# A new order of expert groups and of the last products, with the carried state updated on VectorE

## What is computed

```
C = f_stab * C + i_stab * outer(v_t, k_t);   n = f_stab * n + i_stab * k_t
y_t = sigmoid(o_t) * (C @ q_t) / max(|n . q_t|, 1)
x = y, heads side by side, 1536 x 320
out = sum over 4 experts e of  p[:, e] * (relu(x @ w1[e]) @ w2[e])     # 320 -> 1024 -> 320
```

## Time and profile before

| | |
|---|---|
| median of 3 runs | 412.25 us |
| the profiled execution, its own time | 412.83 us |
| span of its profile | 410.9 us |
| mean granted clock of TensorE | 0.996 of full |
| instructions | 7284 |
| busy: TensorE / VectorE / ScalarE / GpSimd | 403.0 / 261.8 / 192.0 / 193.2 us |
| idle of TensorE in the span | 7.9 us |

### The profile page before, as it was taken

One profiled execution on the slowest core, in us unless ns is written; L12 is line 12 of the kernel. 1 busy time (PEld: TensorE's weight loads), 2 busy tenths in 40 slices (PEclk: granted clock), 3 DMA queues, 4 the chain that ended last, 5 costly groups with the idle time before them and its releaser, 6 DMA issues.

```text
span 410.9 us, 7284 instructions
## 1 busy us (share of the span) xinstructions
PE 403.0 (98%) x2650; PEld 389.8 (95%) x2650; DVE 261.8 (64%) x490; ACT 192.0 (47%) x378; POOL 193.2 (47%) x227
## 2 busy tenths in 40 slices
PE   8999999999899999999999999999999999999997
PEld 8899999999899999999999999979999999999997
DVE  5885786759444538346249893668665666667654
ACT  4575478659242548434125442344553345434420
POOL 4865835487940558821602001567435643556300
PEclk9999999999899999999999999999999999999999
DMA  7889929684970606341016002222012211230002
GB/s 265 283 283 391 381 92 346 234 284 159 369 274 2 225 2 228 116 176 48 2 30 140 0 2 83 85 84 85 12 73 83 83 29 57 83 101 17 0 2 96
DMA packets 18052, 54.48 MB, mean 133 GB/s; under 512 B 2177, under 2 KB 8850, under 8 KB 16866
## 3 DMA queue, kind: packets, MB, share of 16 engines
q1 hardware_dynamic: 17442, 52.63, 36.8%
q10 hardware_dynamic: 576, 1.40, 1.0%
HBM read 50.40 MB, written 2.05 MB: 128 GB/s over the span
## 4 chain that ended last, share of the span: by engine, by line
PE 94%; DVE 4%; issue 1%; ACT 0%; POOL 0%; DVEq 0%
PE acc_ps L1611 21%; PE hid_ps L1592 21%; PE acc_ps L1677 16%; PE out_ps L1548 5%; PE hid_ps L1677 3%; PE acc_ps L1592 2%; PE out_ps L1655 2%; PE out_ps L1656 2%; PE out_ps L1654 2%; PE out_ps L1653 2%; PE out_ps L1555 2%; PE hid_ps L1441 1%; PE score_ps L1492 1%; PE score_ps L1655 1%; PE add_ps L1655 1%; PE add_ps L1656 1%
## 5 line engine op out<-in xcount | busy, mean ns | idle before, releaser
L1149 DVE SCALAR_TENSOR_TENSOR h_lo<-hid_ps,h_hi 128x384 fp32r<-128x384 f32 (+1 forms) x70 | 35.9, 513 | 84.6 <-ACT h_hi L809 84.3
L809 ACT ACTIVATE h_hi<-hid_ps 128x384 fp32r<-128x384 f32 (+1 forms) x70 | 31.8, 455 | 108.6 <-PE hid_ps L1592 108.5
L1611 PE MATMUL acc_ps<-w_hi,h_hi 128*128 128x320 f32 x208 | 66.4, 319 | 2.5 <-DVE y_acc L1169 2.2
L1611 PE MATMUL acc_ps<-w_hi,h_lo 128*128 128x320 f32 x208 | 64.4, 310 | 0.0
L1611 PE MATMUL acc_ps<-w_lo,h_hi 128*128 128x320 f32 x208 | 64.2, 308 | 0.0
L1592 PE MATMUL hid_ps<-xt_hi,w_hi 128*128 128x384 f32 (+1 forms) x210 | 57.1, 326 | 0.1
L1592 PE MATMUL hid_ps<-xt_hi,w_lo 128*128 128x384 f32 (+1 forms) x210 | 56.6, 324 | 0.0
L612 POOL TENSOR_TENSOR w_lo<-w_raw,w_hi 128x384 fp32r<-128x384 f32 x40 | 45.1, 1131 | 23.5 <-ACT w_hi L795 23.4
L682 POOL TENSOR_TENSOR w_hi<-w_raw,w_hi 128x640 fp32r<-128x640 f32 x12 | 19.6, 1634 | 53.1 <-ACT w_hi L852 53.1
L1611 PEld LDWEIGHTS acc_ps<-w_hi,h_hi 128*128 128x128 f32 x208 | 39.5, 190 | 2.8 <-DVE h_lo L1149 2.7
L676 POOL TENSOR_TENSOR left_lo<-w_raw,left_hi 128x384 fp32r<-128x384 f32 x12 | 13.2, 1101 | 56.6 <-ACT left_hi L835 56.6
(11 more groups left out here) (251 smaller groups left out, 996.6 us busy)
## 6 DMA issues: line engine op xcount, KB each, us to landing
w_raw<-in_w_b SPq DMA_DIRECT2D x19, 704.0 KB, 7.3
w_raw<-in_w_s SPq DMA_DIRECT2D x12, 832.0 KB, 4.6
raw<-in_qk_s SPq DMA_DIRECT2D x8, 1024.0 KB
g_all<-g_dram SPq DMA_DIRECT2D x10, 512.0 KB, 6.9
kv<-in_kv_n SPq DMA_DIRECT2D x12, 352.0 KB, 6.1
q_pack<-in_q_p SPq DMA_DIRECT2D x10, 192.0 KB, 6.9
out_y<-y_acc SPq DMA_DIRECT2D x12, 160.0 KB, 1.8
carry<-g_dram SPq DMA_DIRECT2D x30, 60.0 KB
```

The lines of the kernel that those rows point to most:

```text
L809: nc.scalar.activation(h_hi[:, M % RING, 0:cols], hid_bank(M)[:, 0:cols], ACT.Relu).then_inc(hid_hi, 1)
L1149: nc.vector.scalar_tensor_tensor(h_lo[:, M % RING, 0:cols], hid_bank(M)[:, 0:cols], 0.0, h_hi[:, M % RING, 0:cols].bitcast(fp32), ALU.max, ...
L1611: last = nc.tensor.matmul(acc_ps[t][:, 0:DM], x, w, start=(f == 0 and i == 0), stop=(f == NF - 1 and i == 2))
```

## The change

The second and third visit of the first expert are swapped with the third expert (`LOADS`, `GROUPS`): expert 2 meets units 0 to 5 in slots 24 to 39 (three units at a time), and expert 0 meets units 2 and 3 in slots 40 to 47. `EARLY` drops to 24, `DN_END` to 24, and the start slots of units 5 to 10 and the slots of `CAST` and `SUB` move. `carry_state` leaves GpSimd's queue and becomes three `scalar_tensor_tensor` operations of VectorE on 120x123 elements, in the same slot T0+6. In the wide steps, step 1 gets the order 1, 6, 7, 4, 2, 5, 3 with its four downs behind the second, third, fourth and sixth product, the last step gets 4 ahead of 2, and ScalarE and VectorE are reordered to match; `step_rest_low` of the next step moves ahead of the second `add_wide` in every step.

```diff
--- before.py
+++ after.py
@@ -29,16 +29,16 @@
 LAG, FIRST = 2, 4
 EARLY_SPLITS = {M: [M + 4] for M in range(12)}
 
-LOADS = (0, 1, 0, 2, 3)
-GROUPS = ((0, 0, 2), (1, 0, 2), (1, 2, 2), (2, 2, 2), (3, 0, 3), (3, 3, 3), (4, 0, 3), (4, 3, 3), (4, 6, 3), (4, 9, 3))
+LOADS = (0, 1, 2, 0, 3)
+GROUPS = ((0, 0, 2), (1, 0, 2), (1, 2, 2), (2, 0, 3), (2, 3, 3), (3, 2, 2), (4, 0, 3), (4, 3, 3), (4, 6, 3), (4, 9, 3))
 SLOTS = NF * len(GROUPS)
 N_BLOCKS = NF * len(LOADS)
 N_PAIRS = N_BLOCKS // 2
-T0 = {2: 2, 3: 6, 4: 16, 5: 22, 6: 30, 7: 34, 8: 40, 9: 46, 10: 50, 11: 56}
-EARLY = 32
-DN_FIRST, DN_END = 0, 28
-CAST = {4: (11, 12), 5: (16, 17), 6: (24, 25), 7: (28, 30), 8: (35, 37), 9: (41, 43), 10: (44, 47), 11: (51, 52)}
-SUB = {4: (13, 14), 5: (18, 19), 6: (26, 27), 7: (30, 32), 8: (37, 38), 9: (43, 45), 10: (46, 48), 11: (53, 54)}
+T0 = {2: 2, 3: 6, 4: 16, 5: 20, 6: 26, 7: 32, 8: 36, 9: 48, 10: 52, 11: 56}
+EARLY = 24
+DN_FIRST, DN_END = (0, 24)
+CAST = {4: (9, 11), 5: (16, 17), 6: (21, 24), 7: (28, 29), 8: (33, 34), 9: (43, 44), 10: (47, 49), 11: (51, 53)}
+SUB = {4: (13, 14), 5: (18, 19), 6: (23, 25), 7: (29, 30), 8: (34, 35), 9: (45, 46), 10: (49, 51), 11: (53, 54)}
 OPEN_IN = {3: (2,), 13: (4,), 14: (6,), 17: (8,), 18: (10,)}
 LATER_PAIRS = {12: 8, 14: 9, 16: 10}
 
@@ -52,11 +52,15 @@
 SUM_AT = 2 * DM + 4 * 256
 W_STEP = SUM_AT + 4 * 256
 ORDER = (1, 6, 5, 7, 2, 4, 3)
+SECOND_ORDER, LAST_ORDER = (1, 6, 7, 4, 2, 5, 3), (1, 6, 5, 7, 4, 2, 3)
+SECOND_DOWNS = (1, 2, 3, 5)
 LEFT = {1: 0, 2: 1, 4: 2, 5: 3, 6: 4, 7: 5, 3: 6}
 RIGHT = {1: 0, 2: 1, 3: 2, 5: 3, 6: 4, 7: 5, 4: 6}
 TURNED = {5: 0, 7: 1, 4: 2, 6: 3}
 BEGIN = 73
 W_RING = 4
+AT_HEADS = 5
+AT_STATE = 6
 
 
 def group_of(M):
@@ -178,9 +182,19 @@
     return wide_evictions(p - 2, 1, min(i, pairs(p - 2) - 1))
 
 
+def order_of(t):
+
+    return {1: SECOND_ORDER, STEPS - 1: LAST_ORDER}.get(t, ORDER)
+
+
+def blocks_of(t):
+
+    return (21, 11, 12, 22) if t in (1, STEPS - 1) else (11, 21, 12, 22)
+
+
 def product_count(t, m):
 
-    return len(ORDER) * t + ORDER.index(m) + 1
+    return len(ORDER) * t + order_of(t).index(m) + 1
 
 
 def halves_of(t):
@@ -322,7 +336,7 @@
         kv_ones, unit_step, first_in = sem("kv_ones"), sem("unit_step"), [sem(f"first_in{i}") for i in range(B)]
         carry_ready, qs_ready, kw_ready = sem("carry_ready"), sem("qs_ready"), sem("kw_ready")
         cast_done, sub_done = sem("cast_done"), sem("sub_done")
-        fresh_ready, state_scaled, state_ready = sem("fresh_ready"), sem("state_scaled"), sem("state_ready")
+        fresh_ready, state_ready = sem("fresh_ready"), sem("state_ready")
         gate_begun, parts_set, g_high, g_low = sem("gate_begun"), sem("parts_set"), sem("g_high"), sem("g_low")
         floor_ready, den_ready, rden_ready = sem("floor_ready"), sem("den_ready"), sem("rden_ready")
         gated = sem("gated")
@@ -624,19 +638,6 @@
                 q = q_pack[0:KS, kept(k), :, :]
                 nc.gpsimd.tensor_tensor(q, q, carry[:, kept(k), :, :], ALU.mult).then_inc(qs_ready, 1)
 
-            def carry_state(k):
-
-                pool.wait_ge(fresh_ready, k + 1)
-                pool.wait_ge(out_done, k + 1)
-                pool.wait_ge(decay_step, 3)
-                pool.wait_ge(pool_init, 3)
-                st = state[0:KS, kept(k), :].rearrange("p (g c) -> p g c", g=GROUP)
-                nc.gpsimd.tensor_tensor(st, st, decay[:, k - B, :].unsqueeze(2).broadcast_to([KS, GROUP, GROUP * DA]),
-                                        ALU.mult).then_inc(state_scaled, 1)
-                pool.wait_ge(state_scaled, k - B + 1)
-                nc.gpsimd.tensor_tensor(state[0:KS, kept(k), :], state[0:KS, kept(k), :], fresh[:, :], ALU.add)\
-                    .then_inc(state_ready, 1)
-
             def unit_steps():
 
 
@@ -715,8 +716,6 @@
                         weigh_keys(k)
                 if (k := unit_at(M, 2)) is not None:
                     scale_q(k)
-                if (k := unit_at(M, 6)) is not None and k < NT - B:
-                    carry_state(k)
                 for w in blocks_to_split(M):
                     split_low(w)
                 if M in (59, 61):
@@ -949,21 +948,25 @@
                     wide_relu(0, 21)
             keep_1(1)
             wide_relu(0, 12)
-            for t in range(1, STEPS):
-                if t > 1:
-                    keep_1(t)
+            own_highs(2)
+            sums_highs(2)
+            wide_relu(0, 22)
+            step_down_high(2)
+            wide_relu(1, 21)
+            wide_relu(1, 11)
+            keep_5(1)
+            wide_relu(1, 12)
+            wide_relu(1, 22)
+            for t in range(2, STEPS):
+                keep_1(t)
                 if t + 1 < STEPS:
                     own_highs(t + 1)
                     sums_highs(t + 1)
                 keep_5(t)
-                if t == 1:
-                    wide_relu(0, 22)
                 if t + 1 < STEPS:
                     step_down_high(t + 1)
-                wide_relu(t, 11)
-                wide_relu(t, 21)
-                wide_relu(t, 12)
-                wide_relu(t, 22)
+                for c in blocks_of(t):
+                    wide_relu(t, c)
 
 
         @block.vector
@@ -1130,6 +1133,17 @@
                 nc.vector.tensor_tensor(target, add_bank.get(k, add_ps)[0:KS, 0:H * DA],
                                         head_mask[:, :, :, :].rearrange("p g r e -> p (g r e)")[:, 0:H * DA],
                                         ALU.mult).then_inc(fresh_ready, 1)
+
+            def carry_state(k):
+
+                dve.wait_ge(fresh_ready, k + 1)
+                dve.wait_ge(out_done, k + 1)
+                dve.wait_ge(pool_init, 3)
+                for g in range(GROUP):
+                    st = state[0:KS, kept(k), g * GROUP * DA:(g + 1) * GROUP * DA]
+                    last = nc.vector.scalar_tensor_tensor(st, st, decay[:, k - B, g:g + 1], fresh[:, g * GROUP * DA:(g + 1) * GROUP * DA],
+                                                          ALU.mult, ALU.add)
+                last.then_inc(state_ready, 1)
 
             def xt_low(k):
 
@@ -1286,6 +1300,7 @@
 
                 dve.wait_ge(product_done, product_count(t, 6))
                 dve.wait_ge(kept_1_done, t + 1)
+                wait_if(dve, whole_of[12], t)
                 n = width(t)
                 nc.vector.tensor_tensor(sum_2[:, 0:n], out_ps[:, 0:n], kept_1[:, 0:n], ALU.add).then_inc(sum_2_done, 1)
 
@@ -1352,8 +1367,10 @@
                     probs(k, 1)
                 for k, t in taken_in(SUB, M):
                     subtract_high(k, t)
-                if (k := unit_at(M, 5)) is not None and k < NT - B:
+                if (k := unit_at(M, AT_HEADS)) is not None and k < NT - B:
                     keep_heads(k)
+                if (k := unit_at(M, AT_STATE)) is not None and k < NT - B:
+                    carry_state(k)
                 if M == SLOTS - 1:
                     add_expert(M // NF, (0,))
                     wide_low(0, 21)
@@ -1401,23 +1418,36 @@
                 if M == 78:
                     wide_low(0, 11)
             add_12(0)
+            add_2(1)
             wide_low(0, 12)
-            for t in range(1, STEPS):
+            add_3(1)
+            sums_lows(2)
+            add_21(1)
+            wide_low(0, 22)
+            wide_low(1, 21)
+            wide_low(1, 11)
+            step_rest_low(2)
+            add_12(1)
+            wide_low(1, 12)
+            wide_low(1, 22)
+            for t in range(2, STEPS):
                 add_wide(t, 0)
                 add_2(t)
                 if t + 1 < STEPS:
                     sums_lows(t + 1)
+                    step_rest_low(t + 1)
                 add_wide(t, 1)
-                if t + 1 < STEPS:
-                    step_rest_low(t + 1)
-                if t == 1:
-                    wide_low(0, 22)
                 add_3(t)
                 add_wide(t, 2)
-                add_wide(t, 3)
-                wide_low(t, 11)
-                add_21(t)
-                wide_low(t, 21)
+                if t < STEPS - 1:
+                    add_wide(t, 3)
+                    wide_low(t, 11)
+                    add_21(t)
+                    wide_low(t, 21)
+                else:
+                    add_21(t)
+                    wide_low(t, 21)
+                    wide_low(t, 11)
                 add_12(t)
                 wide_low(t, 12)
                 wide_low(t, 22)
@@ -1733,11 +1763,13 @@
             for t in range(1, STEPS + 2):
                 ahead, behind = halves_of(t)
                 turns = [(half_of, i) for half_of in (ahead, behind) if half_of is not None for i in range(pairs(half_of[1]))]
+                at = SECOND_DOWNS if t == 1 else range(len(turns))
                 for n in range(8):
                     if t < STEPS and n < len(ORDER):
-                        product(t, ORDER[n])
-                    if n < len(turns):
-                        wide_down(*turns[n][0], turns[n][1])
```

(4 more changed lines are left out.)

## The result

The changed kernel took **410.35 us** (median of 5 runs, 409.40 to 410.71), the kernel before 413.10 (median of 5 beside it, 412.14 to 414.05): a ratio of **0.9933, 95% interval 0.9909 to 0.9956**. It is faster, by 2.8 us where 5.1 were forecast. The profiled execution took 410.71 us with a span of 409.0.

What follows compares the result with a forecast made beforehand. TensorE, busy 403.0 of 410.9 us, was taken as the bound, so only stalls and slow clock could be won. 4.2 + 0.7 + 0.5 - 0.3 = 5.1 us off 412.83 gave 407.7, forecast as a 407.2 us median, range 406.3 to 410.6.

Steps and rivals of the forecast that it cites:

- New groups and slots: Middle unit slots: TensorE's stalls of 2.2 and 0.3 us at slots 32 and 30 go, with 1.7 of slow clock: 4.2 us.
- new small stalls: Slot 24's boundary and slots 40 to 47 together: small TensorE waits priced at 0.3 us, bounds 0 and 3 us.
- slot 24 boundary: From two-unit to three-unit group: TensorE has 4.05 us of cover for 3.2 us of other engines' work, 0.8 to spare.
- clock stretch: From 106 to 110 us, behind slot 32's stall: granted clock 0.57 of full, costing 1.7 us; forecast to go.
- The carry on VectorE: Three operations a unit at T0+6, taken as 0.9 us; bounds nothing and 2.9 us; GpSimd loses about 16 us of work.
- the rule that was set against this part: Shared SBUF interface: every carry beside a GpSimd split costs 2.9 us, slot 24 stalls about 2 us, sum 2 us smaller.
- Down remainders to GpSimd: Blocks 24 to 27: four operations move from VectorE to GpSimd, each at most 1.13 us there, at no cost.
- Slots 40 to 47: Two units, one slot ahead: ScalarE needs 2.29 against 1.84 us in slots 43 and 44, 0.9 behind against 0.8 spare.
- rival C: Slots 40 to 47: relu chain fails in every slot, 0.8 us of wait each; slower, 415 us; chance 0.08.
- Wide step 1: End of step 1: wait of 0.64 us and its refill go, 0.88, less 0.2 at products 7 and 4: 0.7 us.
- The last step: Behind the last product: 0.24 us wait goes and 54 downs take 7.92 instead of 8.17 us; gain 0.5 us.
- Rival A: Stall of 1 to 2 us moves to slot 24 or the 40s, VectorE's fullness the cause: 408.2 to 411.0 us; chance 0.27.

Runs made afterwards that it cites:

- b1: Only the new tables (groups and unit slots) put into the kernel before: 408.23 us, ratio 0.9888 to the kernel before.
- b3: Only the new order of products and downs in step 1 and the last step put into the kernel before: 412.16 us, ratio 0.9982.
- c4: The kernel before, old tables and order, with the carry on VectorE, its addend from PSUM and one slot earlier than the change: 411.82 us, ratio 0.9977.
- a2: The changed kernel with the carry back on GpSimd: 407.83 us, ratio 0.9879 to the kernel before.
- a3: The changed kernel with the carry's addend kept in PSUM and the carry one slot earlier: 407.69 us, ratio 0.9862 to the kernel before.
- c2: The changed kernel with the carry's addend from PSUM, each carry in the change's own slot: 410.51 us, ratio 0.9951 to the kernel before.
- c1: a3 with one accumulator eviction moved ahead of two VectorE splits at the end of the last step: 407.52 us, ratio 0.9879 to the kernel before.
- c3: The changed kernel with each carry one slot earlier, its addend still in SBUF: 413.13 us, ratio 1.0007 to the kernel before.
- a1: The changed kernel timed and profiled once more, nothing altered: 409.84 us, ratio 0.9925 to the kernel before.
- a4: The changed kernel with only unit 8's carry moved from slot 42 to slot 50: 408.93 us, ratio 0.9885 to the kernel before.

## Why the prediction was right or wrong

**The middle, right in mechanism, a little small.** New groups and slots were priced at 4.2 us with 0.3 of new small stalls; b1 has 4.7 alone, with no stall between A and B. The working of the slot 24 boundary held: with 0.8 us to spare TensorE did not wait in b1. Of the 4.2, 1.7 were the clock stretch, and b3 shows that this part is a matter of the execution: it was there in the profile of before, and in another trace with the same stall it was not. A profile of before without it would have had 186.73 - 1.54 = 185.19, and the tables' gain 3.2. It was right to count most of it for the median all the same, since 44 of 64 executions of the kernel before have a mean clock of 0.996 or less, and one of twelve of the changed kernel; the prediction did not ask how often. By either trace the tables give more than the waits and the clock that were counted, 0.5 us and 0.7; 0.24 of it are the slower downs behind the 2.2 us (1.55 against 1.31 in b3), a refill that the prediction counted at wide step 1 and not here. The rest is not accounted for. One part of the mechanism is not borne out: that the carry at the head of GpSimd's queue, with the late mask behind it, had a share in the stall. Without it there the waits stay (c4, with the carry's short instructions on VectorE instead), and with it there under the new tables there are none (b1, a2).

**The carry on VectorE: the step that failed.** The prediction took 0.9 us a unit, hidden, between bounds of 0 and 2.9. It is 0.35 us an instruction only where GpSimd is idle when it starts, and up to 1.13 beside GpSimd's instructions: 3.02 us for unit 8's three, 1.98 for unit 4's. The upper bound, scaled from the longest L1116, was the right value for the worst unit, and it was set aside on the sentence that GpSimd "has little or evenly spread work" in slots 26, 32, 38 and 42. No row was read for that; in slot 42 GpSimd splits weights without a pause. On TensorE this is the 1.87 us of a2: 1.44 at slot 43, for which the prediction had no sum of its own, since it looked at the boundary of slot 24 and at ScalarE in the 40s and had a carry there only in the bound of 3 us, and 0.43 at slot 24, where "inside the 0.8 us to spare nearly whole" was said of 0.9 us and not of 1.98. In the slots of the 40s ups are one slot ahead, so `h_lo` has 0.8 us to spare; 3.02 us ahead of it can't be hidden, and 1.2 us of them became a wait.

By the rule that was set against this part (the Trainium skill, GPSIMD Engine Reference, section 1, Specifications, on the SBUF interface shared with VectorE) every carry beside a split would be slow and the sum 2 us smaller. The runs agree with both: 1.87 us, and with one tensor in PSUM instead of SBUF the lengthening is gone (a3, c2). The paragraph expected that stall at slot 24; it came mostly at slot 43.

**Down remainders to GpSimd: nothing**, as said: b1 has them, and its one wait for a remainder (0.4 us, at 31 us) lies before all of them.

**Slots 40 to 47.** ScalarE was the worry of the prediction, and of rival C. It made TensorE wait nowhere there: b1 and a2, with the casts in the same slots, have no such row. C fell.

**Wide step 1: 0.7 forecast, 0.45 measured** (by a mark between the steps, 31.25 us before and 30.80 after). The wait and the refill went as worked out. The products behind a single down, in the chain of the changed kernel:

```profile
264.76 0.88 PE acc_ps L1707 x6
265.64 0.40 PE out_ps L1683
...
267.62 0.41 PE out_ps L1683
...
272.34 0.30 PE add_ps L1683
```

A first piece of a product is 0.23 us when nothing is waited for. Products 7 and 4 lost 0.17 and 0.18, where 0.1 each was forecast, and product 3 lost 0.07, for which there was no term. 0.88 less 0.42 is the 0.45 measured.

**The last step: 0.5 forecast, 0.05 measured** (0.50 from B to C, less 0.45). The reader of the earlier trace rows finds this in its place:

```profile
397.94 0.58 DVE add_ps L1325
...
398.54 0.50 ACT w_lo L883
...
399.07 1.02 DVE g_lo L1331 x2
400.09 0.47 DVE y_acc L1343
...
400.70 5.53 PE acc_ps L1707 x36
```

Block 21 was done earlier, as said, and the first 18 downs now run at once behind the last product. The other 36 need an accumulator whose eviction stands on VectorE behind the two `g_lo` pieces. The prediction asked when the operands would be ready, and not when the accumulator would be free. c1 moves this one eviction and gets 0.38 us, which shows it.

**The sum.** 4.7 (tables) - 1.87 (carry) + 0.45 + 0.05 = 3.3 us against 5.1, all of it seen in the traces; the start of the profiled execution took 1.4 of it. The medians give 2.8 with an interval from 1.8 to 3.8. Rival A (a stall moves and shrinks, 408.2 to 411.0) is what happened, in the 40s and without a slow stretch. Its reason, VectorE's fullness, may well be that of the old stall (c4 leaves it where it was), but it was not what the carry cost: c4 puts the same work on VectorE into the fuller old slots and is no slower than before. The forecast's chance of faster (0.82) was borne out and the range held the time.

**Open.** Why a wait of 0.8 us was followed by a slow stretch in the traces of c2, and one of 1.6 us in c3, while those of 1.2 us in the changed kernel and of 2.2 us in b3 were not. It was not tried to spread GpSimd's splits so that they miss the carry.

## What to carry to other kernels

When small work moves from GpSimd to VectorE, and reads both its tensors from SBUF, price it at what VectorE takes *beside* GpSimd's instructions, unless the timeline shows GpSimd idle at that very slot. In these traces that price is what is left of the GpSimd instruction running at the start, up to about 1 us for each instruction; the spread between the shortest and the longest of a like instruction tells of it. If one operand can be left in PSUM, the work keeps its short time, but look at who wants that bank next: a slot too late costs as much as it saved. And when operands come earlier at the end of a chain, look for the buffer's eviction before the gain is booked.

Of all kernels, a3 and c1 are the fastest, at 407.69 and 407.52 us: new tables and order, the carry on VectorE out of PSUM, one slot earlier. a2, with the carry left on GpSimd, takes 407.83 and can't be told from them. Moving the carry as such is worth nothing here once the tables are right.

## What the runs showed of the hardware

- A `scalar_tensor_tensor` of VectorE on 120x123 with both tensors in SBUF takes 0.33 us alone and up to 1.13 (a1) or 1.18 us (c3) beside a GpSimd split. With one tensor in PSUM it never took over 0.345 us in 96 instructions (a3, c1, c2, c4), 64 of them of this width and 32 of 82 columns.
- The long ones wait for GpSimd: in both traces of the changed kernel 11 of 24 took over 0.4 us, and each ended 0.14 to 0.15 us after a GpSimd instruction that was running when it started. So 3.3 to 3.5 is no fixed factor, and the bound scaled by 1.32/0.47 = 2.8 came near by the length of the splits. In slot 42 three in a row met one split each and took 1.13, 0.97 and 1.09 us.
- The same stall of 2.2 us is followed by a granted clock of 0.57 over 4 us in one execution, and by 1.00 in another. Of the kernel before, 44 of 64 executions have a mean clock that tells of a stretch of this size. What one profile shows of it belongs in the sum only by how often it comes, and whole in the range.
- Between two traces of the same kernel the start differs by 1.6 us (mark A at 72.17 and 70.55), which is over half of what this change gains. From A to B and from B to C these two agree within 0.02 us. That is not a rule: from unit 4's to unit 6's outputs a4 took 0.27 us longer with the same code, and the kernel before 1.54 longer than b3.
